# Second half of a two-matrix layer recomputed with seven-product units; last output tile split in two

## The reference

```python
attn_out = _attn_ref(q, k, v, M_prev, z_prev, beta)       # 2 x 8 heads, 576 x 64
x = attn_out.transpose(0, 2, 1, 3).reshape(1152, 512)
# first layer (moe): w_in 512 x 2048, w_out 2048 x 512
h = x @ w_in
x = (np.maximum(h, 0) + np.log1p(np.exp(-np.abs(h)))) @ w_out     # softplus
# second layer (moe2): 8 experts, w1[e] 512 x 1024, w2[e] 1024 x 512
P = gate(x @ w_gate)           # exp, then 8 rounds of row and column scaling
out = sum(P[:, e:e+1] * (np.maximum(x @ w1[e], 0) @ w2[e]) for e in range(8))
```

## Time and profile before

| | |
|---|---|
| times of three runs | 1105.96, 1106.75, 1107.00 us (median 1106.75) |
| profiled execution | 1105.96 us, span of the trace 1104.1 us |
| granted clock of TensorE, mean | 0.998 of full |
| PE / PEld busy | 1091.8 us (99%) / 998.9 us (90%) |
| DVE / ACT / POOL busy | 757.8 us (69%) / 480.8 us (44%) / 443.4 us (40%) |
| chain that ended last | PE 95%, DVE 2%, issue 1%, SPq 1%, POOL 1% |
| attention until about | 139 us |
| first layer, 48 steps | to 341 us, then the logits to 349 us |
| experts | to the end |

### The profile page before, as it was taken

How to read it: one execution, slowest core, us unless ns; L and a number is a source line. 1 busy time by engine, 2 the same in 40 slices (tenths; PEclk the granted TensorE clock), 3 DMA queues, 4 the chain that set the end, 5 groups by cost and what they waited for, 6 DMA issues and landing times.

```text
span 1104.1 us, 19794 instructions
## 1 busy us (share of the span) xinstructions
PE 1091.8 (99%) x6692; PEld 998.9 (90%) x6692; DVE 757.8 (69%) x1329; ACT 480.8 (44%) x1071; POOL 443.4 (40%) x486
## 2 busy tenths in 40 slices
PE   7999999999999999999999999999999999999998
PEld 5888999999997889899899899999999898998997
DVE  7999643453277888776766768667676677767664
ACT  5998764664565233433333333233233232333331
POOL 7899600001044424342443525425343353424420
PEclk9999999999999999999999999999999999999999
DMA  5444202001001110110201111110111102102002
GB/s 124 102 97 102 82 16 77 0 23 56 0 20 39 39 58 20 58 58 20 73 22 57 31 45 57 38 57 19 57 57 37 58 19 57 57 19 68 10 1 86
DMA packets 65924, 52.86 MB, mean 48 GB/s; under 512 B 32464, under 2 KB 53968, under 8 KB 65872
## 3 DMA queue, kind: packets, MB, share of 16 engines
q1 hardware_dynamic: 64672, 51.93, 15.2%
q10 hardware_dynamic: 1200, 0.27, 0.1%
HBM read 49.83 MB, written 2.36 MB: 47 GB/s over the span
## 4 chain that ended last, share of the span: by engine, by line
PE 95%; DVE 2%; issue 1%; SPq 1%; POOL 1%; ACT 0%; DMA 0%; POOLq 0%; ACTq 0%
PE ps_y L1561 40%; PE ps_h L1561 32%; PE ps_g L1561 13%; PE ps_o L1561 4%; PE ps_p L1606 2%; PE ps_s L1580 2%; DVE acc L1429 1%; PE ps_s L1561 0%; PE ps_y L1801 0%; PE ps_t L1533 0%; PE ps_t L1545 0%; DMA raw<-in_moe_w_in_dram 0%; PE ps_g L1801 0%; PE ps_t L1538 0%; DVE zl L1309 0%
## 5 line engine op out<-in xcount | busy, mean ns | idle before, releaser
L690 POOL TENSOR_TENSOR h<-u,p 128x256 f32<-128x256 f32 (+1 forms) x64 | 56.9, 888 | 423.9 <-DVE u L1286 423.9
L1309 DVE SCALAR_TENSOR_TENSOR zl<-h,zh 128x256 fp32r<-128x256 f32 (+1 forms) x256 | 202.6, 809 | 7.2 <-ACT zh L947 7.2
L1561 PE MATMUL ps_y<-w2c_h,zh 128*128 128x512 f32 x512 | 200.3, 391 | 0.0
L1561 PE MATMUL ps_y<-w2c_l,zh 128*128 128x512 f32 x512 | 199.6, 390 | 0.0
L1561 PE MATMUL ps_y<-w2c_h,zl 128*128 128x512 f32 x512 | 199.3, 389 | 0.0
L947 ACT ACTIVATE zh<-h 128x256 fp32r<-128x256 f32 (+1 forms) x256 | 107.1, 442 | 137.5 <-POOL h L690 58.5
L746 ACT ACTIVATE s<-ps_h 128x256 f32<-128x256 f32 (+1 forms) x64 | 26.3, 411 | 289.4 <-PE ps_h L1561 289.4
L1561 PEld LDWEIGHTS ps_y<-w2c_h,zl 128*128 128x128 f32 x512 | 96.1, 188 | 20.3
L1561 PEld LDWEIGHTS ps_y<-w2c_h,zh 128*128 128x128 f32 x512 | 96.2, 188 | 19.2
L1561 PEld LDWEIGHTS ps_y<-w2c_l,zh 128*128 128x128 f32 x512 | 96.2, 188 | 18.6
L1561 PE MATMUL ps_h<-xbh,w1c_h 128*128 128x320 f32 x320 | 98.9, 309 | 0.0
(11 more groups left out here) (251 smaller groups left out, 2969.9 us busy)
## 6 DMA issues: line engine op xcount, KB each, us to landing
rc<-in_moe_w_dram SPq DMA_DIRECT2D x64, 512.0 KB, 3.7
out_dram<-acc SPq DMA_DIRECT2D x9, 256.0 KB, 2.0
q_nat<-in_q_dram SPq DMA_DIRECT2D x16, 128.0 KB, 2.6
...
```

The lines of the kernel that those rows point to most:

```text
L690: pool.tensor_tensor(h22[:, 0:n], u3[:, 0:n], p5[:, 0:n], ALU.add).then_inc(h22_done, 1)
L1309: dve.scalar_tensor_tensor(out=z_place(u, quarter, 1), in0=rows[:, 0:n], scalar=0.0, in1=z_place(u, quarter, 0).bitcast(F32), op0=ALU.max, ...
L1561: last = pe.matmul(dst, a[x], b[y], start=start and i == 0, stop=stop and i == 2)
```

## The change

1. The first 1024 columns of the first layer's width stay plain (`G1 = 1`, 24 steps; the loops over chunks are unrolled). The second 1024 become two halves `s = 0, 1` (`SL = 2`) of four Strassen units each, placed ahead of the experts, which now begin at `s = 2`. The weights come in as the experts' do (`rc1`, `rc2`, 256 columns at a time). The experts' hidden code is used with the first layer's own tokens (`xh`, `xl`).
2. The sums of token quarters that these units need are made from the attention's output. POOL adds high and low part into `x32` (`tokens_whole`, one instruction for 512 tokens, later one for 640), takes four differences (`token_sums`), twice. ACT and DVE split them in chunk 1 (`sums_hi`, `sums_lo`, one per step).
3. Softplus on the units' tiles. Each quarter takes three ACT instructions (`unit_exp_ln`), one DVE (`unit_sum`), one ACT (`unit_hi`) and one DVE (`unit_lo`) in place of relu's one and one. `unit_rest` interleaves them with the drains of output pieces.
4. The output of these units (`output_layer1`) stays transposed and goes in pieces of one bank through five banks; u = 0 and 1 of both halves share an accumulation, and in the first half part of u = 2 and 3. A table (`PIECES`) gives bank, columns and semaphore counts. A piece whose bank is in use waits for its drain.
5. In these eight units POOL, not DVE, makes the low halves of the plain weight quarters (`weights_lo`).
6. At the border to the experts POOL makes the 640-token sums after the last drain, and only then the low halves of the next weights and the results of the first expert unit.
7. The last output tile of the last expert is computed in two halves of 256 columns, each with its own bank, drain and DMA.

```diff
-    G1 = moe_w_in.shape[1] // FS
+    G1, SL = 1, 2
@@ POOL
+            def tokens_whole(t0, n):
+                flat = [...x[:, :, t0:t0 + n] for x in (xh, xl)]
+                pool.tensor_tensor(x32[:, :, 0:n], flat[0].bitcast(F32), flat[1].bitcast(F32), ALU.add)\
+                    .then_inc(x32_done, 1)
...
+            pool.wait_ge(o_lo, G * NP + G)
+            pool.wait_ge(w1_lo, FT)
+            tokens_whole(0, 2 * NA)
+            pool.wait_ge(x32_done, 1)
+            token_sums(x32, 0, NA, xsa, xsa_sum)
+            pool.wait_ge(xsa_sum, 4)
+            tokens_whole(2 * NA, 2 * NB)
+            pool.wait_ge(x32_done, 2)
+            token_sums(x32, 0, NB, xsb, xsb_sum)
             weight_sums(0, 0)
-            pool.wait_ge(y_drained, KT * (C1 + 2) + KT)
-            token_sums(0, NA, xas, xa_sum)
             weight_sums_lo(0, 0)
             weight_sums(0, 1)
+            weight_sums_lo(1, 1)
             result_22(0, 0)
             result_12(0, 0)
-            weight_sums_lo(1, 1)
-            pool.wait_ge(y_drained, KT * G1 * C1 + KT)
-            token_sums(2 * NA, NB, xbs, xb_sum)
+            for s in range(SL):
+                for u in range(4):
+                    U = 4 * s + u
+                    if U + 1 == 4 * SL:
+                        pool.wait_ge(y_drained, Y_ALL)
+                        token_sums(y1, 2 * NA, NB, xbs, xb_sum)
+                    if u >= 2:
+                        weights_lo(2 * s + u, u % 2)
+                        weight_sums_lo(2 * s + u, u % 2)
+                    result_22(U + 1, (u + 1) % 4)
+                    result_12(U + 1, (u + 1) % 4)
...
@@ ACT
+            def unit_exp_ln(U, u, quarter):
+                to = h_work[:, k, 0:width(u)]
+                act.wait_ge(MADE[quarter], U + 1)
+                act.activation(to, ROWS[quarter][:, 0:width(u)], ACT.Abs).then_inc(e_abs, 1)
+                act.wait_ge(e_abs, 4 * U + k + 1)
+                act.activation(to, to, ACT.Exp, scale=-1.0).then_inc(e_exp, 1)
+                act.wait_ge(e_exp, 4 * U + k + 1)
+                act.activation(to, to, ACT.Ln, bias=1.0).then_inc(e_ln, 1)
...
+            act.wait_ge(h_ready, G1 * M1)
+            for part in range(3):
+                weights_hi(0, 1, part)
+            take_s1(0, 0)
+            take_p5(0, 0)
...
+                    take_p5(V, v)
+                    unit_exp_ln(V, v, "11")
+                    unit_exp_ln(V, v, "22")
+                    unit_hi(V, v, "11")
+                    unit_exp_ln(V, v, "12")
+                    unit_hi(V, v, "22")
+                    unit_exp_ln(V, v, "21")
+                    unit_hi(V, v, "12")
+                    unit_hi(V, v, "21")
@@ DVE
+            def unit_sum(U, u, quarter):
+                dve.wait_ge(e_ln, 4 * U + k + 1)
+                dve.scalar_tensor_tensor(out=rows, in0=rows, scalar=0.0, in1=h_work[:, k, 0:n],
+                                         op0=ALU.max, op1=ALU.add).then_inc(e_sp, 1)
...
+            def unit_rest(V, v, drains):
+                for step in (("s", "22"), ("l", "11"), ("s", "12"), ("d",), ("l", "22"), ("d",), ("s", "21"), ("d",),
+                             ("l", "12"), ("d",), ("l", "21"), ("d",), ("d",), ("d",), ("d",)):
...
@@ PE
+            for s in range(SL):
+                for u in range(4):
+                    if 4 * s + u + 1 < 4 * SL:
+                        hidden2(s + (u == 3), (u + 1) % 4, PROD)
+                    output_layer1(s, u)
...
+            hidden2(SL, 0, PROD)
...
+            def last_tile(s):
+                for n, bank in enumerate(LAST_BANKS):
+                    for i in range(2):
+                        for f in range(2):
+                            last = products(bank, (zh[i][:, f, cols], zl[i][:, f, cols]),
+                                            (w2c_h[i][:, f, c], w2c_l[i][:, f, c]), i == 0 and f == 0, i == 1 and f == 1)
```

538 lines of the change are left out of this document (361 added, 177 removed).

## The result

The changed kernel takes 1125.14 us (median of 4 runs, 1124.46 to 1126.54) against 1106.52 us of the kernel before (4 runs on the same chip, 1105.96 to 1107.0): a ratio of 1.017, 95% interval 1.0152 to 1.0188, so 18.6 us slower. The profiled execution has a span of 1122.9 us; before it was 1104.1.

A forecast was written before the change was run, and what follows sets the result against it. PE, busy 99% of the span, was taken as the bound; 1104.1 - 5.0 - 0.3 + 7.5 + 5.1 + 4.8 + 4.1 = 1120.3 us of span, with 1.9 and 0.8 us on top 1123 us, range 1106 to 1131.

The forecast's parts named there:

- the second wait: Plain stage, near 155 us: PE waits about 3 us for DVE's `hl`, held by POOL's second `x32`.
- `s1` at P2: Second unit: product P2 waits 2.3 us for ACT's `s1`, taken only after softplus of the first unit.
- `h21` at the border: Second expert unit: P1 is released by DVE's `h21`, with POOL's list full before it; 4.1 us.
- `u2` at P7 of the first unit: First unit: P7 starts 1.7 us late, released by DVE's `u2` behind a weight split held by POOL.
- PE's own work: Matmuls removed (99.8 us) against matmuls added (94.8 us) in the first layer: a gain of 5.0 us.
- Start of the plain stage: POOL's two `x32` hold DVE's `w2l` and `hl`; PE waits 4.2 and 3.3 us, 7.5 us together, bounds 0 and 11.
- Entry: Entry to the units: PE waits 1.7 us at P7, 1.1 for `h21`, 2.3 for `s1`; 5.1 us, bounds 1.5 and 7.
- Inside: Inside the units: late `s1` before (1,0), bank waits in (0,3) and (1,2), wait before (1,3); 4.8 us, bounds 1 and 9.
- Border: Border to the experts: `h21` waits behind POOL's token sums, low halves and `h22`; PE waits 4.1 us, bounds 1.5 and 7.
- The rival with the clock: Rival on the granted clock: four waits of 3 to 4 us at 1.7 us each, 6.9 us; chance not given.
- The rival in which only the two long instructions bite: Units keep pace, and only POOL's two long `x32` at the plain stage cost time: 1111 us; chance 20%.
- The faster one: Plain stage: `hl` comes through the port while POOL works on `x32`; 1105.4 us, at best 1102; chance 13%.

The follow-up runs named there:

- experiment 1: Kernel before plus only POOL's new work at the start of the plain stage (two `x32`, eight sums, results unused): 1112.98 us, ratio 1.006.
- experiment 6: Changed kernel with DVE's first drain one place earlier in outputs with more than four drains: 1123.89 us, 1.2 less than the changed kernel.
- Experiment 11: Changed kernel with `x32` in pieces, border and drain order edits, and relu for softplus in the units (another function): 1106.35 us, ratio 1.0001 to the kernel before.

## Why the prediction was right, point by point

The forecast was 1123 us with a range of 1106 to 1131; 1125.14 us lies in it, and slower is what it gave 83%. Of the signs that it named, those at the start (the second wait with 0.76 us instead of some 3), `s1` at P2 and `h21` at the border came; `u2` at P7 of the first unit and a lower busy time of PE did not.

- **PE's own work**, -5.0 us: right, -5.2 in two kernels (after, and relu).
- **Start of the plain stage**, 7.5 us: right in mechanism, order and place; 6.6 found, and 6.7 as the whole effect of experiment 1. 4.59 and 6.05 us for `x32` (4.7 and 5.9 foreseen). The step that was off: the second stall of 3.3 us was reckoned from PE at full clock. PE ran at 1.2 GHz for most of 4 us, used up 1.6 us of the stall in that way and stood for 0.76; the rest went with the first `hl`, which came 0.6 us later than walked. A fallen clock cost nothing where a wait would have come anyway.
- **Entry**, 5.1 us: of its three waits 1.1 and 2.3 us are there (0.79 and 2.14, with restarts 3.4), that of 1.7 us at P7 is not. I let POOL's 1024-element half start in the middle of DVE's two weight splits; DVE began them at 242.65 and had both done at 243.67, and POOL, which began at 243.33, held neither. Which engine came first was a matter of 0.7 us.
- **Inside**, 4.8 us: the term that was mis-sized, 7.9 us. (0,3) 1.1 us instead of 1.75, s1 before (1,0) 1.07 instead of 1.15; but 2.53 instead of 0.6 in (1,2). There the walk did not price POOL's four 512-token sums for the experts, which run from 332.92 to 338.69 us: three of DVE's instructions took 1.59, 1.55 and 1.17 us beside them instead of some 0.5, the bank's drain stood behind the first two, and the clock fell there for 1.5 us. The 1.3 us before (1,3) were not paid on top: experiment 6 shows them at 1.28 as soon as the bank wait before them shrinks. One chain of softplus had been counted as two waits. No run moves the token sums alone, so their share is read from the rows and not shown by an edit.
- **Border**, 4.1 us: 3.79 us, plus the clock. The size is right by two errors that cancel: from the last drain to the end of `h21` it was 15.3 us (351.34 to 366.68) instead of 14.2, and PE had 11.5 us of work for it instead of 10.1.
- **The rival with the clock**: it held in part. It counted four waits of 3 to 4 us at 1.7 us each, 6.9 us; two such waits came. Of the waits over 2 us (3.64, 2.14, 2.18, 3.79) three went with a fall; one of those cost nothing, two about 1.5 us each, 3 us together.
- **The rival in which only the two long instructions bite**: out, 11.4 us of waits lie elsewhere. **The faster one**: out by experiment 1, where `w2l` and `hl` again last to the end of `x32`. Experiment 11 shows that even without softplus the saving is spent.

That the sum came out near is in part luck: 1.7 us too much at the entry, 0.9 at the start, against 3.1 too little inside, 1.4 at the border and the attention's 1.0.
